# A delta-rule recurrence with mixing and gated attention on one core: the triangular inverse by doubling with T and M in one product, additions on GpSimd

## The reference

```python
for t in range(S):
    y[:, :, t] = np.einsum('bhd,bhde->bhe', rt, state)
    Sa = np.einsum('bhde,bhe->bhd', state, at)
    state_decay = state * wt[:, :, None, :] - np.einsum('bhd,bhe->bhde', Sa, bt)
    state = state_decay + np.einsum('bhd,bhe->bhde', vt, kt)
```

## Time and profile before

| | |
|---|---|
| median of 3 runs | 1196.84 us (1196.66 to 1200.7) |
| the profiled execution | 1200.26 us |
| its span, first to last instruction | 1198.5 us |
| mean granted TensorE clock | 0.960 |
| PE / PEld busy | 1062.2 us (89%) / 794.6 us (66%), 24816 instructions each |
| DVE / ACT / POOL busy | 539.4 (45%) / 382.9 (32%) / 325.3 us (27%) |

### The profile page before, as it was taken

The page is one execution under the profiler, slowest core; times in us unless marked ns, Lnnn a source line. Parts: engine busy times, 40 slices in busy tenths (PEclk is TensorE's granted clock), DMA queues, the critical chain, the costliest instruction groups (busy, mean ns, idle before and its releaser), DMA issues. The chain is left out here.

```text
span 1198.5 us, 54422 instructions
## 1 busy us (share of the span) xinstructions
PE 1062.2 (89%) x24816; PEld 794.6 (66%) x24816; DVE 539.4 (45%) x1152; ACT 382.9 (32%) x1021; POOL 325.3 (27%) x588
## 2 busy tenths in 40 slices
PE   5777777899999898899999898799999898899978
PEld 4766666766667676666666677676666686655556
DVE  5444444433334766423334586513334676210274
ACT  2322222322112454422212355332212354410155
POOL 4543444322222333112223343212232330000000
PEclk9888889899999999999999999899999999999989
DMA  3534222212111222102111122111221111000000
GB/s 116 153 108 147 82 81 81 81 39 60 46 56 45 80 72 64 54 27 61 39 59 50 54 85 72 50 33 40 58 63 39 44 37 50 26 1 1 1 12 23
DMA packets 47940, 68.57 MB, mean 57 GB/s; under 512 B 19680, under 2 KB 34784, under 8 KB 47712
## 3 DMA queue, kind: packets, MB, share of 16 engines
q1 hardware_dynamic: 47712, 65.08, 18.4%
HBM read 57.19 MB, written 7.86 MB: 54 GB/s over the span
## 5 line engine op out<-in xcount | busy, mean ns | idle before, releaser
L484 POOL TENSOR_TENSOR QI<-R,consts 128x256 f32<-128x256 f32 x240 | 173.9, 735 | 480.2 <-DVE R L653 442.8
L653 DVE COPY R<-PB 128x512 f32<-128x512 f32 x147 | 101.1, 688 | 190.4 <-PE PB L916 188.2
L546 ACT COPY R<-PB 128x512 f32<-128x512 f32 x147 | 86.6, 589 | 238.7 <-PE PB L916 236.9
L908 PEld LDWEIGHTS PB<-R 64*64 64x64 f32 x5376 | 106.5, 143 | 67.8 <-issue 54.0
L908 PE MATMUL PB<-R 64*64 64x64 f32 x5376 | 128.3, 234 | 24.9 <-issue 11.4
L1139 PE MATMUL PB<-uf,W 128*128 128x384 f32 x320 | 112.0, 496 | 1.3 <-ACT ur L597 1.3
L1164 PE MATMUL PB<-work,W 128*128 128x384 f32 x320 | 108.0, 491 | 2.4 <-DVE work L827 2.4
L916 PE MATMUL PB<-R,QI 64*64 64x64 f32 x3072 | 83.4, 230 | 9.6 <-issue 9.3
L1139 PEld LDWEIGHTS PB<-uf,W 128*128 128x128 f32 x320 | 58.0, 190 | 46.6 <-issue 12.7
L1164 PEld LDWEIGHTS PB<-work,W 128*128 128x128 f32 x320 | 59.2, 190 | 42.0 <-issue 2.9
L827 DVE TENSOR_SCALAR work<-PB 128x384 f32<-128x384 f32 x40 | 22.3, 558 | 127.1 <-PE PB L1144 74.5
(11 more groups left out here) (138 smaller groups left out, 1945.7 us busy)
## 6 DMA issues: line engine op xcount, KB each, us to landing
EA<-ea_dram SPq DMA_DIRECT2D x48, 498.0 KB, 3.5
LA<-la_dram SPq DMA_DIRECT2D x48, 384.0 KB, 3.4
VT<-vt_dram SPq DMA_DIRECT2D x48, 80.0 KB, 1.9
x_mid_dram<-XO SPq DMA_DIRECT2D x192, 20.0 KB, 1.9
xs<-x_mid_dram SPq DMA_DIRECT2D x24, 160.0 KB, 2.8
out_dram<-work SPq DMA_DIRECT2D x24, 160.0 KB, 2.1
W<-w_dram SPq DMA_DIRECT2D x1, 1600.0 KB, 11.1
W<-w_dram SPq DMA_DIRECT2D x1, 1280.0 KB, 7.7
```

Of the source, the lines that this page charges most:

```text
L484: nc.gpsimd.tensor_tensor(QI[j][:].rearrange("p (u g t) -> p u g t", u=2, g=2), src.rearrange("p u (g t) -> p u g t", g=2), eye3.unsqueeze ...
L546: freed(nc.scalar.copy(tile[:, 8 * C:16 * C], PB[PLACE[group, i][0]][:, 1, :]), group, i)
L653: freed(nc.vector.tensor_copy(tile[:, 0:8 * C], PB[PLACE[group, i][0]][:, 0, :]), group, i)
L908: mm = nc.tensor.matmul(out[half(m1), u, col:col + C], left, right, start=True, stop=True)
```

## The change

The inverse is now summed: M' = M + Q M. A power's tile holds for each of two heads the columns Q, T and M side by side. One step of `double` makes Q Q with 64 columns, and with the same Q as weights the products for T and M in one matmul of 128 columns. The product QM is added to the old M by GpSimd in place (`add_up`), after the copies; the next round waits for this sum (`m_made`). The last two steps, d4 and d5, take the places of r6 and r7; q5 is the square of r5 alone. The halves of the partitions are put back at each copy: ScalarE copies bank 1 in two operations of 64 partitions, each into the other half. A2 is now copied by both engines: VectorE takes bank 0 and VK, ScalarE bank 1 in two halves. W1, U and V are loaded at the very start, W2 at the first z, the others at the last h of the first batch, each with its own semaphore that TensorE or VectorE waits for where it is first used.

```diff
-        "r1": 0, "r2": 0, "r3": 0, "r4": -1, "r5": -1, "r6": -1, "r7": -2,
+        "r1": 0, "r2": 0, "r3": 0, "r4": -1, "q5": -1, "d4": -1, "d5": -2,
         "U": -2, "X": -2, "ST": -2, "o1": -2, "o2": -3, "o3": -3, "s1": 2, "s2": 1, "s3": 1}
-MEMBERS = {"A1": ("r4", "r7"), "A2": ("r1",), "A3": ("U", "o2"),
-           "B1": ("r2", "r5"), "B2": ("X", "o3"), "B3": ("s2", "s1"),
-           "C1": ("r3", "r6"), "C2": ("s3", "ST"), "C3": ("o1",)}
+MEMBERS = {"A1": ("r4", "d5"), "A2": ("r1",), "A3": ("U", "o2"),
+           "B1": ("r2", "q5"), "B2": ("X", "o3"), "B3": ("s2", "s1"),
+           "C1": ("r3", "d4"), "C2": ("s3", "ST"), "C3": ("o1",)}
...
-        if what in ("A1", "A2", "B1", "C1"):
-            return 2
+        if what in ("A1", "B1", "C1"):
+            return 3
+        if what == "A2":
+            return 4
...
-        R1, R25, R36, R47 = sb("R1", [P, 8 * C]), sb("R25", [P, 16 * C]), sb("R36", [P, 16 * C]), sb("R47", [P, 16 * C])
+        R1 = sb("R1", [P, 2, 6 * C])
+        R25, R36, R47 = (sb(name, [P, 2, 8 * C]) for name in ("R25", "R36", "R47"))
         VK = ring("VK", VK_DEPTH, TOK)
-        M1 = sb("M1", [P, 4 * C])
-        QI = {k: sb(f"QI{k}", [P, 4 * C]) for k in range(1, 6)}
...
+        def sums(tile):
+            return tile[:, :, 0:6 * C].rearrange("p u (g x t) -> p u g x t", g=2, x=3)[:, :, :, 2, :]
+
+        def pairs(tile):
+            return tile[:].rearrange("p u (g c) -> p u g c", g=2)[:, :, :, 0:2 * C]
+
+        def in_pairs(ps):
+            return ps[:, :, 0:4 * C].rearrange("p u (g c) -> p u g c", g=2)
+
+        def last_two(tile):
+            return tile[:, :, 6 * C:8 * C].rearrange("p u (g t) -> p u g t", g=2)
...
-            def load_weights(part):
...
-                elif part == 2:
...
+            def load_wide(dst, src, sem_):
+                sp.dma_start(dst[:, 0:2, :], t[src][0:2 * P, :].rearrange("(f p) n -> p f n", p=P)).then_inc(sem_, 16)
+                for j in range(2):
+                    sp.dma_start(dst[half(j), 2, :], t[src][2 * P:DM, :]).then_inc(sem_, 16)
+
+            load_wide(W1, "w1", w1_in)
+            sp.dma_start(Uw[:], t["U"].rearrange("(s p) r -> p s r", p=P)).then_inc(uv_in, 16)
+            for j in range(P // RK):
+                sp.dma_start(Vw[j * RK:(j + 1) * RK, :], t["V"]).then_inc(uv_in, 16)
...
+                elif (what, i, *args) == ("z", 0):
+                    sp.dma_start(W2[:], t["w2"].rearrange("(m p) n -> p m n", p=P)).then_inc(w2_in, 16)
+                elif (what, i, *args) == ("h", 0, NM - 1):
+                    load_wide(WVG, "wvg", wvg_in)
+                    load_wide(WK, "wk", wqk_in)
+                    load_wide(WQ, "wq", wqk_in)
+                    sp.dma_start(hide[:], t["cst"][:, 0:P]).then_inc(rest_in, 16)
+                    sp.dma_start(tie[:], t["cst"][:, P:P + E * E]).then_inc(rest_in, 16)
+                    sp.dma_start(WO[:], t["wo"].rearrange("(j p) n -> p j n", p=P)).then_inc(rest_in, 16)
...
-            def make_qi(j, n, tile, lo):
-                taken(pool, f"r{j}", n)
-                src = tile[:].rearrange("p (u c) -> p u c", u=2)[:, :, lo:lo + 2 * C]
-                nc.gpsimd.tensor_tensor(QI[j][:].rearrange("p (u g t) -> p u g t", u=2, g=2),
-                                        src.rearrange("p u (g t) -> p u g t", g=2),
-                                        eye3.unsqueeze(1).to_broadcast([P, 2, 2, C]), ALU.add
-                                        ).then_inc(qi_made[j], 1)
+            def add_up(j, what, n, here, before):
+                taken(pool, what, n)
+                nc.gpsimd.tensor_tensor(here, here, before, ALU.add).then_inc(m_made[j], 1)
+                pool.wait_ge(m_made[j], n + 1)
...
-                nc.gpsimd.tensor_tensor(gt(M1[:, 0:2 * C]), gt(UP[:, 0:2 * C]), eye3.to_broadcast([P, 2, C]), ALU.add
-                                        ).then_inc(m1_made, 1)
-                for p in range(2):
-                    pool.wait_ge(m1_made, 3 * n + 1 + p)
-                    nc.gpsimd.tensor_tensor(gt(M1[half(1 - p), 2 * C:4 * C]), gt(UP[half(p), 4 * C:6 * C]),
-                                            eye3[half(p)].to_broadcast([C, 2, C]), ALU.add).then_inc(m1_made, 1)
-                pool.wait_ge(m1_made, 3 * n + 3)
+                nc.gpsimd.tensor_tensor(sums(R1), UP[:].rearrange("p (u x g t) -> p u x g t", u=2, x=2, g=2)[:, :, 0],
+                                        eye3.unsqueeze(1).to_broadcast([P, 2, 2, C]), ALU.add).then_inc(m_made[1], 1)
+                pool.wait_ge(m_made[1], n + 1)
...
-                elif what == "A1" and chunk_of("r4", i) is not None:
...
+                elif what == "A1":
+                    if chunk_of("d5", i) is not None:
+                        add_up(6, "d5", chunk_of("d5", i), last_two(R47), last_two(R36))
+                    if chunk_of("r4", i) is not None:
+                        add_up(4, "r4", chunk_of("r4", i), sums(R47), sums(R36))
+                elif what == "B1" and chunk_of("r2", i) is not None:
+                    add_up(2, "r2", chunk_of("r2", i), sums(R25), sums(R1))
                 elif what == "den":
                     make_den(i + LEAD["den"])
-                elif what == "C1" and chunk_of("r3", i) is not None:
-                    make_qi(3, chunk_of("r3", i), R36, 0)
+                elif what == "C1":
+                    if chunk_of("r3", i) is not None:
+                        add_up(3, "r3", chunk_of("r3", i), sums(R36), sums(R25))
+                    if chunk_of("d4", i) is not None:
+                        add_up(5, "d4", chunk_of("d4", i), last_two(R36), sums(R47))
...
-                freed(nc.scalar.copy(tile[:, 8 * C:16 * C], PB[PLACE[group, i][0]][:, 1, :]), group, i)
+                for p in range(2):
+                    freed(nc.scalar.copy(tile[half(p), 1, :], PB[PLACE[group, i][0]][half(1 - p), 1, :]), group, i)
...
-                    freed(nc.scalar.copy(R1[:].rearrange("p (u c) -> p u c", u=2), ps[:, :, 0:4 * C]), "A2", n)
-                    freed(nc.scalar.copy(at(VK, n)[:], ps[:, 0, 4 * C:4 * C + TOK]), "A2", n)
+                    for p in range(2):
+                        freed(nc.scalar.copy(pairs(R1)[half(p), 1], in_pairs(ps)[half(1 - p), 1]), "A2", n)
...
+                elif what == "A2":
+                    is_full(dve, "A2", n)
+                    ps = PB[PLACE["A2", n][0]]
+                    freed(nc.vector.tensor_copy(pairs(R1)[:, 0], in_pairs(ps)[:, 0]), "A2", n)
+                    freed(nc.vector.tensor_copy(at(VK, n)[:], ps[:, 0, 4 * C:4 * C + TOK]), "A2", n)
...
-            def square(j, out, to, R, lo, both_=True):
...
-                        mm = nc.tensor.matmul(out[half(m1), u, col:col + C], left, right, start=True, stop=True)
-                return mm
-
-            def extend(j, out, to, M, lo):
-                per = M.shape[1] // 2
+            def double(out, R):
                 for g, p, u in HEADS:
-                    m0 = p ^ (u * (j % 2))
-                    m1 = m0 ^ u
-                    mm = nc.tensor.matmul(out[half(m1), u, to + g * C:to + g * C + C],
-                                          QI[j][half(m0), u * 2 * C + g * C:u * 2 * C + g * C + C],
-                                          M[half(m0), u * per + lo + g * C:u * per + lo + g * C + C],
-                                          start=True, stop=True)
+                    lo = 3 * g * C
+                    nc.tensor.matmul(out[half(p ^ u), u, lo:lo + C], R[half(p), u, lo + C:lo + 2 * C],
+                                     R[half(p), u, lo:lo + C], start=True, stop=True)
+                for g, p, u in HEADS:
+                    lo = 3 * g * C
+                    mm = nc.tensor.matmul(out[half(p ^ u), u, lo + C:lo + 3 * C], R[half(p), u, lo:lo + C],
+                                          R[half(p), u, lo + C:lo + 3 * C], start=True, stop=True)
...
-                return square(2, out, 0, R1, 0)
+                pe.wait_ge(m_made[1], n + 1)
+                return double(out, R1)
 
             def round3(n, out):
                 taken(pe, "r2", n)
-                square(3, out, 0, R25, 0)
-                pe.wait_ge(m1_made, 3 * n + 3)
-                pe.wait_ge(qi_made[1], n + 1)
-                return extend(1, out, 4 * C, M1, 0)
+                pe.wait_ge(m_made[2], n + 1)
+                return double(out, R25)
 
             def round4(n, out):
                 taken(pe, "r3", n)
-                square(4, out, 0, R36, 0)
-                pe.wait_ge(qi_made[2], n + 1)
-                return extend(2, out, 4 * C, R36, 4 * C)
-
-            def round5(n, out):
+                pe.wait_ge(m_made[3], n + 1)
+                return double(out, R36)
+
+            def fifth_square(n, out):
                 taken(pe, "r4", n)
-                square(5, out, 4 * C, R47, 0, False)
-                pe.wait_ge(qi_made[3], n + 1)
-                return extend(3, out, 6 * C, R47, 4 * C)
-
-            def round6(n, out):
```

(35 more changed lines are left out.)

86 lines of the change are left out of this document (32 added, 54 removed).

## The result

The changed kernel takes 1204.4 us (median of 20 runs, 1197.6 to 1210.22), the kernel before on the same chip 1200.76 us (20 runs, 1192.6 to 1210.36): a ratio of 1.005, interval 1.003 to 1.0071. Executions more than 1.5% above the fastest of their kernel are left out of this and all later ratios. The forecast was 1203 us, or 6.1 us more than the 1196.84 of three runs; against the 20 runs the change costs 3.6 us by the medians and 6 by the ratio. Its profiled execution has a span of 1202.4 us. I read it by the same views as before.

What follows compares the result with a forecast made beforehand. TensorE was taken as bound by instruction delivery alone and by its own order beside mixing. Terms -17 + 0 + 13.3 + 12.8 - 2 - 1 = +6.1 us on 1196.84 gave 1203 us, range 1181 to 1225.

Steps and rivals of the forecast that it cites:

- alone, inverse: Recurrence-alone stage: fewer TensorE instructions save 23 us, less 6 for waits on drains and sums; 17 us saved, bounds 0 and 23.
- weights: Moved weight loads: some 4 us saved in the alone stage, 3 us added in mixing; -1 us, bounds -4 and +4.
- mixing, halves: Beside mixing, ScalarE's two half copies hold A3, C3 and B3: 0.70 us a round, 19 rounds, +13.3 us.
- array: TensorE's array beside mixing and attention: a 128-column product takes 30 ns, twice a 64-column one's 15; nothing gained.
- attention: Beside attention, ScalarE's half copies hold TensorE: 0.6 or 1.2 us a round, +12.8 us, between 3 and 22.
- issue waits of over 0.4 us after the first stage: TensorE waits no semaphore explains, after 231.7 us: ten, 9.7 us together; a tenth fewer instructions give -2 us.
- last batch: The stage after the recurrence has ended: no term in the forecast's sum, so 0.
- The rival in which the stage gives nothing: Alone stage: the chain of copies and additions takes the place of instruction fetch, no gain; 1220 us, chance 0.16.
- a second operation starts 0.48 us after one of 512 columns: ScalarE's half copies: second starts 0.48 us after the first and lasts 0.59; drain ends 1.13 us after the last product.
- Neither rival on columns: Products of 128 columns: dear at 34 ns, 1209 us, chance 0.10; or cheap at 23 ns, 1192 us, chance 0.07.
- The rival with the drains covered there: Beside attention softmax waits cover the drains, costing only 3 us, and the alone stage gives all 23; 1184 us, chance 0.28.

Runs made afterwards that it cites:

- e11: The kernel before itself, unchanged, profiled and timed a second time: ratio 1.0006 to the kernel before.
- e5: Changed kernel meant to get 96 empty instructions a round; they are not in the profiled program, so it is a second measurement of the changed kernel: 1202.75 us.
- e10: Changed kernel with the weights loaded at chunks 2 to 8, as in the kernel before: 1207.68 us, ratio 1.0048 to the kernel before.
- e2: Kernel before with only the weights' loads and their waits moved as in the change: 1191.41 us, ratio 0.9917 to the kernel before.
- e7: Second run of the kernel before with only the weights' loads and their waits moved: 1188.62 us, ratio 0.9857 to the kernel before.
- e1: Changed kernel with ScalarE's two half copies of A1, B1, C1 and A2 made one; halves not exchanged, values differ from the reference's: 1167.22 us.
- e4: Changed kernel with each product of 128 columns issued as two of 64, 96 instructions more a round: 1231.9 us, ratio 1.0275 to the kernel before.
- e6: Changed kernel with single ScalarE copies that keep the halves; two DMAs move the bank-1 sum to the other half: 1193.79 us, ratio 0.9932 to the kernel before.
- e9: Chunks 0 to 13 as in the changed kernel, later ones with single copies and the old sum moved by DMA: 1174.49 us, ratio 0.979 to the kernel before.
- e3: Chunks 0 to 13 with the changed inverse, later ones with the old inverse and single copies, weights moved: 1191.21 us, ratio 0.9903 to the kernel before.

## Why the prediction was right, and where it was not

The total, 1203 against 1204.4 us, was right, and so was its shape: a gain alone, given back beside mixing and attention by ScalarE's halves. That it came so close is in part luck. The first z came 25 us earlier (means of two profiles) where the sum had 21, and the weights' 3 us in mixing did not come; against that the halves cost 3 to 4 us more in mixing than I gave them. These errors offset each other in part: by the stages of the profiles the change costs 2 us, by the ratio 6. The terms, against the means of the profiles of before and e11 and of the changed kernel and e5 where nothing else is named:

| term | forecast | measured |
|---|---|---|
| alone, inverse | -17 | -22 (e10 against before), -18 (changed against e2 and e7) |
| weights | -4 alone, +3 in mixing | -3 alone (changed against e10), 0 in mixing |
| mixing, halves | +13.3 | +16.5, and +17.6 against e1 |
| array | 0 | about 0 |
| attention | +12.8 | +9.6 (with most of the next row in it), and +12.3 against e1 |
| issue waits of over 0.4 us after the first stage | -2 | -5 and -7 (9.7 us before, 5.0 and 3.1 in the changed kernel and e5) |
| last batch | 0 | +1 |

*Alone.* The account by blocks held: e4 put a block at 4.1 us where I had used 4.26. The waits for GpSimd's sums came to 6.1 us; I had given some 6 to them and to A2's drain together. The stage ended at 207 and not near 213 us, and one thing there the forecast left out: with fewer waits the granted clock was 0.96 and not 0.88. How much of the gain is the clock's, no run separates. The "issue" waits of the earlier trace rows are 36 and not 33, which changes no term. The rival in which the stage gives nothing is out. The rule of the Trainium skill ("Runtime: NRT & Kernel Launch", Instruction fetch mechanics), that such crossings are mostly hidden, holds beside mixing, where e4's extra pairs cost 1.1 and 0.4 us in two of three stages (the other, 7.5 us longer, stays unexplained), and fails alone, where they cost 22.7 us.

*Halves beside mixing.* The mechanism was right, the size too small: 0.87 to 0.93 us a round over 19 rounds, and not 0.70. The step that failed is "a second operation starts 0.48 us after one of 512 columns". I had read that from a whole copy followed by an exponential from another bank. Two half copies follow each other without overlap, 1.18 us together and not 1.07, so that TensorE starts 1.31 us after the group's end at A3, at C3, and at B3 too (267.42 to 268.73), where I had counted 0.07.

It isn't the bank that makes the difference. Here are two whole copies of the kernel before that both read bank 0 of one PSUM tile; then, of the changed kernel, two half copies and behind them a whole one of another tile:

```profile
67.88 0.59 ACT L571 COPY R<-PB 128x512 f32<-128x512 f32 x1 [0.56 <-PE PB L934]
68.36 0.30 ACT L572 COPY VK<-PB 128x160 f32<-128x160 f32 x1
...
66.62 1.18 ACT L556 COPY R<-PB 64x512 f32<-64x512 f32 x2 [2.62 <-PE PB L961]
67.83 0.29 ACT L586 COPY XS<-PB 128x160 f32<-128x160 f32 x1
```

L572 starts 0.1 us before L571 ends, as it does in all 48 chunks. In all 147 pairs of half copies of the changed kernel the second starts 0.02 to 0.03 us after the first has ended, and L586 does so behind them too. Whether that is due to the 64 partitions or to the change of halves, no run separates.

*Array.* 27.5 ns a wide pair, at the lower bound of 28; I took 30. Neither rival on columns is left: 34 ns would be 0.54 us for sixteen, 23 ns 0.37, and it is 0.44.

*Attention.* The forecast sum was right, but the length of the stages can't prove it alone: two profiles of each kernel spread over 3 to 6 us. e1, e6 and e9 have 310.0 to 312.0 us with single copies, the four profiles with halves 321.5 to 330.9; but e3, with single copies too, has 323.0, at a low clock. What carries it are the waits: TensorE's waits for ScalarE's copies of these groups (of over 0.15 us) are 18.0 and 18.5 us in the changed kernel and e5, and 3.2 in the kernel before, 3.4 in e3 and 3.6 in e1; VK's copy, ScalarE's too in the old inverse, adds 1.9 and 1.5 us before and in e3. The rival with the drains covered there is out by that. All of TensorE's waits there together grew by less, from 47 to 54 us, since some only take the place of others.

*Weights.* Measured where the forecast speaks, in the changed kernel, it was right (1.0048 and 1.005). That the same edit is worth 0.8 to 1.4% to the old kernel was outside my bounds. What I had as its mechanism, the wait of 4.6 us, is gone in e2 and e7 (longest 2.5 and 2.7 us), but the sum of waits has hardly changed. And e11, where W2 is loaded as before, has no wait of over 2.1 us either, and 1.6 us where W2 lands; e10 has 4.0 us there. So the size of that wait belonged to one execution, and it can't be taken as the price of the load.

## What to carry to other kernels

Where TensorE is fed with many small products and is idle for part of the time, count instructions; where its own order is the bound, count only what lies between a group's last product and its drain's end. An edit that saves the one and lengthens the other belongs only in the stage where TensorE is idle in part: here a switch by chunk number (e9) turned +0.5% into -2.1%. And when only a small part of a result has to change partitions, move that part beside the path rather than the whole on it.

## What the runs showed of the hardware

- Half the partitions save nothing of a copy's time: 580 ns for 64x512 on ScalarE, 588 for 128x512. Fewer columns do: on GpSimd an addition of 128x128 took 0.46 us and one of 128x256 0.73.
- On ScalarE whole copies that follow each other overlap by 0.1 us (L571 and L572 of the kernel before), half copies that change halves do not.
- With small products a block of 256 instructions took 3.6 to 4.1 us in the windows shown of the stage alone, whether TensorE was busy 2.3 or 3.5 us of them, and 6.5 to 8.0 us while W2 was landing (before, e11, e10).
- The granted clock differs between executions of one kernel, and the time with it: of 73 executions of the kernel before, the eight with a mean clock of 0.967 to 0.971 took 1191.23 to 1199.17 us, twelve with 0.949 to 0.953 took 1204.9 to 1213.49. In one place that I looked at it fell after a lull of TensorE, in the changed kernel (windows beside attention):

```profile
742.00:744.00 2.00, 0.51 (x11) 0.45 (x4) 1.88 (x5) 0.32 (x2) 0.74 (x2) 0.97 0.00 0
744.00:746.00 2.00, 1.34 (x30) 0.94 (x32) 1.93 (x5) 0.57 (x2) 1.62 (x3) 0.50 0.16 41
746.00:748.00 2.00, 2.00 (x34) 1.88 (x28) 0.98 (x2) 0.87 (x2) 0.00 (x0) 0.50 0.55 146
```

TensorE was busy 0.51 of 2 us at a mean clock of 0.97; then it worked at 0.50, the lower of its two levels, 1.2 GHz, in the last window without a gap.
